# A first step rebuilt: products on VectorE, summed in PSUM by transposing, and the last rows of the previous partition in four transfers

## The reference

```
w = exp(weight_gen - max);  w = w / (sum(w) + 1e-09)
out = einsum('bshk,bskhg->bshg', w, x_unf)       # x_unf: 7 shifted copies of x, 192 wide
h = out @ w_in                                    # 192 -> 2048
g = s * relu(h)**2 + b
result = g @ w_out                                # 2048 -> 192
```

## Time and profile before

| | us |
|---|---|
| median of 3 runs (lowest to highest) | 1178.69 (1177.63 to 1178.88) |
| the profiled execution, whole | 1179.33 |
| its span, first to last instruction | 1177.4 |
| TensorE busy in the span | 1148.5 |
| VectorE, ScalarE, GpSimd busy | 910.5, 780.6, 149.0 |

### The profile page before, as it was taken

The page is one execution under the profiler, slowest core; times in us unless marked ns, Lnnn a source line. Parts: engine busy times, 40 slices in busy tenths (PEclk is TensorE's granted clock), DMA queues, the critical chain, the costliest instruction groups (busy, mean ns, idle before and its releaser), DMA issues.

```text
span 1177.4 us, 32125 instructions
## 1 busy us (share of the span) xinstructions
PE 1148.5 (98%) x13216; PEld 1046.2 (89%) x13216; DVE 910.5 (77%) x1162; ACT 780.6 (66%) x844; POOL 149.0 (13%) x97
## 2 busy tenths in 40 slices
PE   3799999999999999999999999999999999999998
PEld 3799999999998999998999999999999999999997
DVE  6977778877778877778877778877779777779743
ACT  3466666776666776666776666776666676667674
POOL 7401110011110011110011110111110111110111
PEclk8899999999999999999999999999999999999999
DMA  6111101111101111101111101111101111101000
GB/s 181 39 39 51 51 13 37 51 51 51 51 13 37 51 51 51 51 13 37 51 51 51 51 13 37 51 51 51 42 22 37 51 51 51 36 22 43 14 14 28
DMA packets 18409, 51.06 MB, mean 43 GB/s; under 512 B 2140, under 2 KB 9691, under 8 KB 18394
## 3 DMA queue, kind: packets, MB, share of 16 engines
q1 hardware_dynamic: 18245, 50.27, 12.6%
q10 hardware_dynamic: 149, 0.59, 0.2%
HBM read 38.27 MB, written 12.58 MB: 43 GB/s over the span
## 4 chain that ended last, share of the span: by engine, by line
PE 96%; DVE 2%; POOL 1%; DMA 1%; ACT 0%; issue 0%; ACTq 0%; DVEq 0%; POOLq 0%
PE hp L670 44%; PE op L692 35%; PE op L700 15%; PE hp L630 1%; DVE g_lo L547 1%; DMA x_in<-in_x 1%; POOL tap_pool L324 0%; POOL acc L333 0%; PE hp L636 0%; DVE g_hi L543 0%; DVE x_in L196 0%; DVE acc L500 0%; DVE tap L500 0%; DVE out_sb L563 0%; DVE out_sums L559 0%
## 5 line engine op out<-in xcount | busy, mean ns | idle before, releaser
L692 PE MATMUL op<-wo,g_hi 64*128 64x384 f32 x4096 | 609.0, 360 | 5.5 <-DVE g_lo L547 5.5
L700 PE MATMUL op<-wo,g_lo 64*128 64x192 f32 x4096 | 514.2, 248 | 0.0
L670 PE MATMUL hp<-xT,w_hi 64*128 64x512 f32 x3072 | 480.1, 390 | 3.1 <-ACT r L393 1.9
L393 ACT ACTIVATE r<-hp 128x1024 f32<-128x1024 f32 x256 | 257.4, 1019 | 322.7 <-PE hp L670 320.4
L692 PEld LDWEIGHTS op<-wo,g_hi 64*128 64x128 f32 x4096 | 386.1, 185 | 15.0 <-DVE g_lo L547 6.1
L700 PEld LDWEIGHTS op<-wo,g_lo 64*128 64x128 f32 x4096 | 392.6, 188 | 5.4
L547 DVE TENSOR_TENSOR g_lo<-r,g_hi 128x1024 fp32r<-128x1024 f32 x256 | 315.8, 1234 | 50.7 <-ACT g_hi L404 43.6
L670 PEld LDWEIGHTS hp<-xT,w_hi 64*128 64x128 f32 x3072 | 279.2, 185 | 59.3 <-ACT r L393 1.8
L670 PE MATMUL hp<-xT,w_lo 64*128 64x512 f32 x1536 | 303.7, 392 | 0.0
L397 ACT ACTIVATE r<-r 128x1024 f32<-128x1024 f32 x256 | 271.1, 1059 | 6.9
L500 DVE TENSOR_TENSOR tap<-x_in,w_soft 128x768 f32<-128x768 f32 (+1 forms) x192 | 184.0, 959 | 3.3
(11 more groups left out here) (42 smaller groups left out, 276.2 us busy)
## 6 DMA issues: line engine op xcount, KB each, us to landing
x_in<-in_x SPq DMA_DIRECT2D x30, 960.0 KB, 4.9
out<-out_sb SPq DMA_DIRECT2D x31, 384.0 KB, 2.3
w_in<-in_weight_gen SPq DMA_DIRECT2D x32, 112.0 KB, 2.0
wo_raw<-in_moe_w_out SPq DMA_DIRECT2D x4, 384.0 KB, 7.5
w_raw<-in_moe_w_in SPq DMA_DIRECT2D x4, 256.0 KB, 5.5
x_in<-in_x SPq DMA_DIRECT2D x1, 768.0 KB, 7.0
x_in<-in_x ACTq DMA_DIRECT2D x1, 540.0 KB
w_raw<-in_moe_w_in SPq DMA_DIRECT2D x8, 64.0 KB, 4.9
```

What stands on the lines that cost most here:

```text
L393: nc.scalar.activation(r[:, b, :], hp[:, PAIR * b:PAIR * (b + 1), :], ACT.Relu).then_inc(relu_done, 1)
L670: mm = nc.tensor.matmul(hp[:, j, :], w, xt, start=start, stop=stop)
L692: nc.tensor.matmul(op[:, t, 0:2 * D], g_hi[rows[h], g % 2, j, t * P:(t + 1) * P], wo[rows[h], k, :, :].rearrange("p a d -> p (a d)"), star ...
L700: mm = nc.tensor.matmul(op[:, t, 0:D], g_lo[rows[h], g % 2, j, t * P:(t + 1) * P], wo[rows[h], k, 0, :], start=False, stop=(k == FT - 1 an ...
```

## The change

In words:

- **Halo.** Both halos come in four transfers, one per batch, of 31 rows each, and none touches the first partition of a batch. The zeroing waits for nothing now: for step 0 two partitions by GpSimd and two by VectorE at the head of their lists, for step 1 all four by GpSimd.
- **Queues.** ScalarE issues the first group of the first weights, SyncE the halo of step 0 behind `x`. SyncE's order changes: group 1 of the first weights and group 0 of the second before the inputs of step 1, the rest after it.
- **Tokens of step 0.** VectorE makes all seven products of all four tokens, k = 6 first, into `first_taps`; nothing is added on VectorE or GpSimd. TensorE transposes each product and adds the seven in PSUM: 16 transposes to a product, 112 in all. The halo is waited for before the product k = 5.
- **Split of step 0's result.** Columns 64 to 191 are transposed as one block, so the small operand lands in partitions 64 to 127, with one instruction for two on either engine, then a copy.
- **Weights.** GpSimd splits none. VectorE writes all low parts: one group ahead of the first step, the others between its pairs; the last of the second weights in step 1, behind the last two pairs of step 0.
- **Column sums.** In halves of 64 rows into two banks, one part amid the transposes, one behind the first product of group 0, two behind that of group 1. The bias takes two instructions.
- **ScalarE** runs relu of pairs 0 and 1 back to back, and spreads the high parts of the later weights over step 0.

```
         def load_halo(queue, i):
             before = PAD - STEP * i
-            for a, n in ((1, 120), (121, 7)):
+            rows_of_batch = S // TOK
+            for q in range(B):
+                a, n = q * rows_of_batch + 1, rows_of_batch - 1
                 queue.dma_start(x_in[a:a + n, i, 0:before, :], ...
...
             load_w(0)
             load_first_x(0)
-            load_w1(0)
-            for g in range(NG): (wo_raw, group g)
-            load_w1(1)
+            load_halo(sp, 0)
+            load_wo(0)
+            load_w1(sp, 1)
+            sp.wait_ge(w_shifted, 1)
+            load_w(1)
+            load_wo(1)
+            load_first_x(1)
+            load_halo(sp, 1)
+            load_wo(2)
+            load_wo(3)
             sp.dma_start(s_col ...
             sp.dma_start(b_col ...
-            load_w1(2), load_w1(3), load_first_x(1), load_halo(sp, 1)
-            sp.wait_ge(w_shifted, 1)
-            load_w(1)
+            load_w1(sp, 2)
+            load_w1(sp, 3)
...
         @block.scalar
-            load_halo(act, 0)
+            load_w1(act, 0)
...
             hi_of_w1(0)
-            for g in range(NG):
-                hi_of_wo(g)
+            hi_of_wo(0)
             hi_of_w1(1)
-            hi_of_attn(0)
-            hi_of_w1(2)
-            hi_of_w1(3)
+            hi_of_attn(0, first=True)
+            hi_of_wo(1)
             step(0, first=True)
...
+            def first_step_taps():
+                dve.wait_ge(w_soft_ready, 1)
+                dve.wait_ge(x_loaded[0], FETCH)
+                for k in reversed(range(K)):
+                    if k == K - 2:
+                        dve.wait_ge(x_halo_loaded[0], B * FETCH)
+                        dve.wait_ge(pool_zeroed, PAIR)
+                        dve.wait_ge(dve_zeroed, B - PAIR)
+                    nc.vector.tensor_tensor(first_taps[:, k, :, :] ..., x_in[:, 0, k:k + STEP, :] ...,
+                        w_soft[:, :, :, k] ..., ALU.mult).then_inc(tap_ready, 1)
...
+            def first_step():
+                lo_of_attn(0, first=True)
+                lo_of_w1(1)
+                shift_weights(1)
+                lo_of_wo(0)
+                normalise_weights(1)
+                taps(1, 1, range(0, 1), FETCH, halo=True)
+                split_g(0, 0, True)
+                split_g(0, 1, True)
+                bias_of_colsum()
+                lo_of_wo(1)
+                lo_of_w1(2)
+                taps(1, 1, range(1, 5), FETCH, halo=True)
+                split_g(0, 2, True)
+                split_g(0, 3, True)
+                lo_of_wo(2)
+                lo_of_w1(3)
+                taps(1, 1, range(5, K), FETCH, halo=True)
+                split_g(0, 4)
+                split_g(0, 5)
+
+            def step(i, parity, x_count, second=False, last=False):
                 lo_of_attn(i)
                 if not last:
                     shift_weights(i + 1)
+                split_g(i - 1, PAIRS - 2)
+                split_g(i - 1, PAIRS - 1)
+                if second:
+                    lo_of_wo(3)
...
+            def sum_first_attn(k):
+                start, stop = k == K - 1, k == 0
+                pe.wait_ge(tap_ready, K - k)
+                for t in range(STEP):
+                    for h in range(2):
+                        last = nc.tensor.matmul(op[:, h, t * D2:(t + 1) * D2], first_taps[rows[h], k, t, 0:P], ident[rows[h], rows[h]],
+                                                start=start and t == 0, stop=stop and t == STEP - 1, is_transpose=True)
...
+            def column_sums(c):
+                pe.wait_ge(wo_loaded[c], FETCH)
+                for k in range(c * GROUP, (c + 1) * GROUP):
+                    for h in range(2):
+                        mm = nc.tensor.matmul(op[:, 2 + h, 0:D], ones[rows[h], :], wo_raw[rows[h], k, :], ...)
...
                     first_product(i, g, first)
+                    if first and g == 0:
+                        column_sums(1)
                     if g > 0:
                         if first and g == 1:
+                            column_sums(2)
+                            column_sums(3)
                             pe.wait_ge(bias_ready, 1)
...
-            column_sums()
-            pe.wait_ge(sum_ready, K - 1)
-            pe.wait_ge(pool_sum_ready, K - 1)
-            transpose_attn_a()
-            transpose_attn_b()
+            for k in reversed(range(K)):
+                sum_first_attn(k)
+                if k == 3:
+                    column_sums(0)
             step(0, first=True)
             pe.wait_ge(wo_lo_ready, NG)
             with pe.Fori(1, STEPS - 1) as i:
```

More of the change, by code:

```diff
@@ L183, in by_token, with load_w1 @@
             return rows.rearrange("p (u e h c) -> p u e h c", u=STEP // 2, e=2, h=2)[:, :, e, :, :]
+        def load_w1(queue, g):
+            cols = slice(g * GROUP * P, (g + 1) * GROUP * P)
+            queue.dma_start(w1_raw[:, cols], moe_w_in[0:P, cols]).then_inc(w1_loaded[g], FETCH)
+            by_parity = moe_w_in[P:D, cols].rearrange("d (m h c) -> d m h c", h=2, c=P)
+            half_cols = slice(g * PAIR * P, (g + 1) * PAIR * P)
+            for half in range(2):
+                queue.dma_start(w2_raw[half * D2:(half + 1) * D2, half_cols].rearrange("d (m c) -> d m c", c=P),
+                                by_parity[:, :, half, :]).then_inc(w1_loaded[g], FETCH)
         def load_halo(queue, i):
             before = PAD - STEP * i
-            for a, n in ((1, 120), (121, 7)):
+            rows_of_batch = S // TOK
+            for q in range(B):
+                a, n = q * rows_of_batch + 1, rows_of_batch - 1
                 queue.dma_start(x_in[a:a + n, i, 0:before, :],
@@ L277, in _ @@
         def _(pool):
[L280 to L290, removed]
+            for q in range(PAIR):
+                zero_batch_start(nc.gpsimd, 0, q).then_inc(pool_zeroed, 1)
+                pool.wait_ge(pool_zeroed, q + 1)
+            nc.gpsimd.memset(ones[:, :], 1.0).then_inc(pool_step, 1)
+            pool.wait_ge(pool_step, 1)
             nc.gpsimd.affine_select(out=ident[:, :], in_=ones[:, :], compare_op=ALU.is_equal, fill=0.0,
@@ L293, in _ @@
             pool.wait_ge(ident_ready, 1)
[L295 to L348, removed]
+            for q in range(B):
+                zero_batch_start(nc.gpsimd, 1, q).then_inc(pool_zeroed, 1)
+                pool.wait_ge(pool_zeroed, PAIR + q + 1)
             def add_sums(i, first=False):
@@ L419, in step @@
                 for q in range(PAIRS - 1):
-                    relu(i, q, first)
+                    if not (first and q == 1):
+                        relu(i, q, first)
+                    if first and q == 0:
+                        relu(i, 1, first)
                     if q == PAIRS - 2:
@@ L427, in step @@
                         hi_of_g(i, q, first)
+                    if first and q == 1:
+                        hi_of_w1(2)
+                    if first and q == 2:
+                        hi_of_wo(2)
+                    if first and q == 3:
+                        hi_of_w1(3)
+                        hi_of_wo(3)
+                        act.wait_ge(sb_loaded, 2 * FETCH)
                     if q == 1 and not first:
@@ L489, in taps @@
                         dve.wait_ge(x_loaded[parity], x_count)
[L490 to L497, removed]
+                        if halo:
+                            dve.wait_ge(x_halo_loaded[1], B * FETCH)
+                            dve.wait_ge(pool_zeroed, PAIR + B)
+                        else:
+                            dve.wait_ge(sum_ready, sums_before(i))
@@ L569, in bias_of_colsum @@
                 dve.wait_ge(sb_loaded, 2 * FETCH)
-                nc.vector.tensor_scalar(bias[:, :], op[:, 0, 0:D], b_col[:, 0:1], None, ALU.mult).then_inc(bias_ready, 1)
-            def zero_batch_starts(i, batches):
-                dve.wait_ge(x_halo_loaded[i], 2 * FETCH)
-                for q in batches:
-                    zero_batch_start(nc.vector, i, q).then_inc(dve_zeroed, 1)
-            def step(i, parity, x_count, first=False, last=False):
-                halo = first
+                nc.vector.tensor_scalar(scaled_sum[:, :], op[:, 2, 0:D], b_col[:, 0:1], None, ALU.mult).then_inc(sum_scaled, 1)
+                dve.wait_ge(sum_scaled, 1)
+                nc.vector.scalar_tensor_tensor(out=bias[:, :], in0=op[:, 3, 0:D], scalar=b_col[:, 0:1], in1=scaled_sum[:, :],
+                                               op0=ALU.mult, op1=ALU.add).then_inc(bias_ready, 1)
+            def first_step():
[19 more added lines that the diff above has]
+            def step(i, parity, x_count, second=False, last=False):
                 lo_of_attn(i)
@@ L639, in transpose_attn_b @@
                 last.then_inc(t_ready, 1)
+            def sum_first_attn(k):
[5 more added lines that the diff above has]
+                                                start=start and t == 0, stop=stop and t == STEP - 1, is_transpose=True)
+                if stop:
```

(45 more changed lines are left out.)

157 lines of the change are left out of this document (88 added, 69 removed).

## The result

The changed kernel takes 1195.28 us (median of 4 runs, 1194.42 to 1195.92) against 1178.79 us of the kernel before: a ratio of 1.0145, 95% interval 1.013 to 1.016. It is 16.5 us slower; 14.2 were forecast. The profiled execution took 1195.92 us with a span of 1193.9.

The account below looks back on a forecast made before the run. TensorE, busy 98% of the span, was taken as the bound, so only the start of step 1 counts: from 69.06 us to 80.4, worth 83.2 with half clock, +14.2 on 1179.33 gives 1193.5, forecast 1193 us, range 1184 to 1202.

Parts of the forecast that it names:

- The place: Start of step 1, 69.06 us before: TensorE's work from there is untouched, so the change is worth its shift, +14.2 us.
- The halo on one engine: Start of step 0: all four transfers of 31 rows queue on one DMA engine; halo landed at 27.6 us, before 7.6.
- From the halo to the first product: Step 0, halo landing to first product by the weights: six VectorE products 5.7 us, then 2.4 us, reaching 35.7.
- From there to second product 0: Step 0, 35.7 to 49.0 us: first products 0 and 1, column sums, and about 1.1 us for the bias with TensorE waiting.
- VectorE's list: Step 0 after the bias: VectorE decides, with low parts, products, sums and pairs 2 to 5, until about 70.6 us.
- From there to step 1: 70.6 to 80.4 us: TensorE idles 5.4 us for the fourth low part of the second weights, behind pairs 6 and 7.
- the half clock: Start of step 1: after the idle TensorE runs at 1.2 GHz, some 3 us lost, charged as 2.8.
- (1): Halo of step 0: 31 rows spread over 16 engines, landing at about 9.3 us; 1175.5 us, faster; chance 0.12.
- (2): Halo of step 0: one engine per transfer, but four different ones; landing at 11.5 us, about 1177 us; chance 0.06.
- (3): Ahead of step 1: halo on one engine but no stall, VectorE through earlier; 8.2 us less, 1185 us; chance 0.05.
- (4): Halo of step 0: the crowded rate on the one engine, landing at 34 us; 6.4 us more, 1200 us; chance 0.10.
- At nothing: Costs taken as nothing: relu 0 and 1 back to back, spread high parts, GpSimd's step 1 zeroings; also SyncE's added wait.

## Why the prediction was right, point by point

**The place.** That the change is worth what it does to the start of step 1 held: 83.94 + 2.2 - 69.06 = 17.1 us, against 16.6 between the two profiled executions. The half microsecond between them is not placed.

**The halo on one engine** (term: landed at 27.6) was right as a mechanism, shown from both sides: the line put into the kernel before costs 23.7 us, taken out of the changed kernel it gives 20.8, and the closing packets are one to a transfer. All four on the same engine: shown by 6.4% of 16. The landing was 29.97, 2.4 later. The sum had the halo's rows begin at 4.7 us (2.5, and 56 KB ahead of them), run 22.9 us, and land the moment the last byte moved. They began at 5.43, took 23.5 us, and VectorE started 1.06 us behind the last: 0.7, 0.6 and 1.1. Alone a row took 0.18 us, which is the rate of the sum; it took up to 0.36 where the other engines worked too.

**From the halo to the first product** (5.7 + 2.4) was 8.7. The six products took 5.3, but the quarter of the column sums amid the transposes took 2.7, where 1.0 stood in the sum for one; I had costed that part inside a lump of 2.4 and not at the clock of an engine that had just idled. The view gives a clock of 1.00 for that stretch, but the durations speak for half: a set of eight transposes follows the one before by 0.43 us up to 36.7 us, and by 0.25 from 37.1 on.

**From there to second product 0** (13.3) was 14.2: first product 5.0 and the bias 1.0 as forecast, two quarters of column sums 2.76 instead of 2.0. **VectorE's list** up to pair 5 was 20.6 (52.85 to 73.45) instead of 21.6; the terms written for that stretch, 11.9, 2.1, 4.9 and 3.1, give 71.0 and not the 70.6 that the sum used. **From there to step 1** it was 10.5 instead of 9.8, the idle part of it 5.8 instead of 5.4, and **the half clock** cost 2.2 instead of 2.8. Undersized: 2.4, 0.6, 0.9 and 0.7; oversized: 1.0 and 0.6. That nets 3.0, the distance from 83.2 to 86.1. That the total came within 3 us is in part luck: terms of up to 2.4 us were off, and two of them the other way.

**The rivals.** (1) and (2) fell with the packets; (3) fell with the 5.8 us of wait; (4) with 0.18 us a row once the other engines had done. What (1) promised, about 1175.5 us, is what the kernel cut in 16 and 15 gave, 1174.5: the walk behind the halo was priced well, with the same errors in both directions in it.

**"At nothing."** SyncE's added wait cost nothing. But the walk let only a sixteenth of each later load stand behind the halo, and in fact the issuing itself was held for 5 us at a time. It cost nothing that the traces show: behind the halo VectorE waits for no load, and TensorE only for VectorE and ScalarE.

## What to carry to other kernels

In these runs a DMA's row count decided how many engines moved it: before cutting a transfer at a natural border, look whether the pieces still have equal shares over many engines, and read it off by the closing packets of a queue. When work is moved to another engine, look at what it is queued behind there and who waits for it: the 0.95 us of low part cost 8 us by its place alone. Mind the length of a wait and not its sum alone: behind one of 3.7 us, and behind one of 5.8, TensorE lost another 1.6 to 2.9 us at half clock. A bad part of a change can hide good ones; here the early zeroing alone was worth 4.2 us, under a line that cost 21.

## What the runs showed of the hardware that was not expected

- While one engine alone worked off the halo, single issues took 5.4 to 5.8 us, and one on SyncE 14.7 us while the halo was on ScalarE's queue, against 0.4 us otherwise. That a full queue at that engine stops the issuing is my reading; how many entries an engine takes was not measured.
- Cutting 31 rows in 17 and 14 is 13.2 us worse than in 16 and 15.
- Column sums of 16 records took 2.7 us start to start on TensorE after idling, 1.2 us later: a factor of 2.3, where two sets of transposes, 0.43 and 0.25 us, differ by 1.7. In the kernel cut in 16 and 15 the same part took 1.7 us (13.00 to 14.70). Why was not tried.
